# A half-filled token tile in two matmul passes instead of three, on one Trainium2 core

## The reference

```
kv = einsum('bhsd,bhse->bhde', k, v);  out = einsum('bhsd,bhde->bhse', q, kv)
x = out / sqrt(mean(out * out, -1) + 1e-6) * g_norm      # then heads side by side: (B, S, 512)
```

```
q, k, v = x @ wq[e], x @ wk[e], x @ wv[e];  a = softmax(causal(scale * q @ k.T))
ye = a @ v @ wo[e];  out += gate[e] * ye                 # gates: softmax over the top 2 of x @ w_gate
```

```
h = gelu_tanh(x @ w_in);  u, v = h[..., :512], h[..., 512:]
v_n = (v - mean(v)) / sqrt(var(v) + 1e-6) * g_ln
v_s = einsum('ts,bsd->btd', w_sg, v_n) + b_sg[None, :, None]
out = x + (u * v_s) @ w_out
```

## Time and profile before

| | |
|---|---|
| median of 3 runs | 925.42 us (923.89 to 925.64) |
| the profiled execution's own time | 923.37 us |
| its span, first to last instruction | 921.6 us |
| mean granted TensorE clock over it | 1.000 of full |
| busy: PE, PEld | 889.8 us (97%), 765.3 us (83%) |
| busy: DVE, ACT, POOL | 460.2 us (50%), 410.9 us (45%), 176.3 us (19%) |

### The profile page before, as it was taken

How to read it: one execution, slowest core, us unless ns; L and a number is a source line. 1 busy time by engine, 2 the same in 40 slices (tenths; PEclk the granted TensorE clock), 3 DMA queues, 4 the chain that set the end, 5 groups by cost and what they waited for, 6 DMA issues and landing times.

```text
span 921.6 us, 17530 instructions
## 1 busy us (share of the span) xinstructions
PE 889.8 (97%) x7009; PEld 765.3 (83%) x7009; DVE 460.2 (50%) x1218; ACT 410.9 (45%) x971; POOL 176.3 (19%) x209
## 2 busy tenths in 40 slices
PE   7699999999999999999999999999999999999897
PEld 3587898979888798978989789897988879897796
DVE  1667623475345743377334762347534574337730
ACT  0646523473335633365244652347333563336521
POOL 0400233003320033101330023300332003310230
DMA  9930303003030032100230030300303000000001
GB/s 278 268 62 2 97 8 94 10 2 104 6 98 2 1 104 60 44 2 22 84 87 18 1 101 4 95 9 2 104 7 97 2 2 1 20 33 1 1 1 52
DMA packets 77648, 45.76 MB, mean 50 GB/s; under 512 B 54592, under 2 KB 70976, under 8 KB 77568
## 3 DMA queue, kind: packets, MB, share of 16 engines
q1 hardware_dynamic: 77568, 44.63, 18.4%
HBM read 35.19 MB, written 9.44 MB: 48 GB/s over the span
## 4 chain that ended last, share of the span: by engine, by line
PE 81%; DVE 10%; ACT 7%; issue 1%; POOL 0%; DMA 0%; POOLq 0%; ACTq 0%; DVEq 0%
PE w L871 38%; PE t L871 19%; ACT probs L566 5%; PE t L925 4%; PE t L1013 4%; PE w L910 3%; DVE neg_max L686 3%; PE w L1058 3%; DVE probs L707 2%; PE t L941 2%; PE t L1002 2%; PE t L957 2%; PE w L978 2%; PE t L1021 2%; ACT work L579 1%; DVE yT L812 1%
## 5 line engine op out<-in xcount | busy, mean ns | idle before, releaser
L871 PE MATMUL w<-wout_s,big 128*128 128x512 f32 x480 | 119.2, 397 | 1.6 <-DVE big L735 1.6
L871 PE MATMUL w<-wsgT_s,big 128*128 128x288 f32 x768 | 110.8, 300 | 0.0
L871 PE MATMUL t<-big,wqk_s 128*128 128x288 f32 x768 | 109.6, 298 | 0.0
L871 PEld LDWEIGHTS w<-wsgT_s,big 128*128 128x128 f32 x768 | 103.3, 189 | 5.2 <-issue 5.2
L871 PEld LDWEIGHTS w<-wout_s,big 128*128 128x128 f32 x480 | 89.3, 188 | 22.0 <-DVE big L735 2.1
L871 PEld LDWEIGHTS t<-big,wqk_s 128*128 128x128 f32 x768 | 102.8, 188 | 0.4
L566 ACT ACTIVATE probs<-w,neg_max 128x64 f32<-128x64 f32 (+4 forms) x160 | 83.0, 525 | 44.5 <-DVE neg_max L686 44.5
L487 POOL TENSOR_TENSOR var_eps<-bn,eps_t 128x1 f32<-128x1 f32 x40 | 13.3, 333 | 445.6 <-DVE bn L723 444.9
L579 ACT ACTIVATE work<-t 128x384 f32<-128x384 f32 (+3 forms) x160 | 63.1, 448 | 44.5 <-PE t L925 44.1
L837 DVE SCALAR_TENSOR_TENSOR work<-w,gln_c,bias_t 128x576 f32<-128x576 f32 x32 | 26.2, 818 | 111.7 <-PE w L871 111.7
L600 ACT ACTIVATE big<-work 128x576 fp32r<-128x576 f32 x32 | 21.9, 686 | 133.1 <-POOL work L494 133.1
(11 more groups left out here) (104 smaller groups left out, 1417.2 us busy)
## 6 DMA issues: line engine op xcount, KB each, us to landing
kin<-in_k_dram SPq DMA_DIRECT2D x8, 1024.0 KB, 6.4
vin<-in_v_dram SPq DMA_DIRECT2D x8, 1024.0 KB, 9.5
qin<-in_q_dram SPq DMA_DIRECT2D x32, 256.0 KB, 4.8
out_dram<-work SPq DMA_DIRECT2D x32, 256.0 KB, 2.1
staged_win<-in_moe_w_in_dram SPq DMA_DIRECT2D x4, 512.0 KB, 5.7
probs<-in_moe_w_sg_dram SPq DMA_DIRECT2D x4, 288.0 KB, 4.1
kin<-in_k_dram SPq DMA_DIRECT2D x8, 128.0 KB, 3.2
vin<-in_v_dram SPq DMA_DIRECT2D x8, 128.0 KB, 7.4
```

What stands on the lines that cost most here:

```text
L871: last = nc.tensor.matmul(o, stationary(hs, c), mv(hm, c), start=c == of[0] and p == 0, stop=c == of[-1] and p == len(PASSES) - 1)
```

## The change

Where the first token tile is the stationary operand, its padding columns now hold the LO parts of the same 64 tokens (HI, columns 0 to 63). Two passes, (HI, HI) and (HI, LO), then give in result rows 64 to 127 the products of the high parts, and in rows 0 to 63 those of the low parts; the sum of the two halves is the product. ACT copies rows 0 to 63 down into partitions 64 to 127 (`low_v`, `low_h`, `low_out`), and DVE adds rows 64 to 127 to that. The four matmul groups lose their third pass.

With it go: DVE writes the LO part of tile 0 into the padding of HI, as an instruction of its own (in `xT`, `yT` and the gated tile `big2`); rows 0 to 63 of `vals` are set to zero once by POOL; an entry `low` for `h` 0 stands ahead of `h` 1 in the list, so that its sum is taken down at once, and `gelu` 0 works in place on the sum; and `h` 1 now takes the narrow buffers' turn, while `h` 2 goes to w1.

```diff
-    MLP = [("pv", N - 3), ("t", N - 2), ("h", 0), ("h", 1), ("scale", N - 1), ("t2", N - 2), ("gelu", 0), ("gelu", 1),
+    MLP = [("pv", N - 3), ("t", N - 2), ("h", 0), ("low", 0), ("h", 1), ("scale", N - 1), ("t2", N - 2), ("gelu", 0), ("gelu", 1),
-    H_SLOT = {1: "w1", 3: "w0", 4: "t1"}
+    H_SLOT = {2: "w1", 3: "w0", 4: "t1"}
...
+        low_v = sq_tile[:, 0:VW]
+        low_h = ln_tile[1]
+        low_out = probs[:, 0, 0, PAD:PAD + 512]
...
+                    elif U == ("v", 0):
+                        nc.scalar.activation(low_v[PAD:P, :], src(U)[0:PAD, 0:VW], ACT.Copy).then_inc(low_v_ready, 1)
                     elif kind == "v":
+                        if j == 1:
+                            u.wait_drained(act, part, i, ("v", 0))
+                    elif kind == "low":
+                        nc.scalar.activation(low_h[PAD:P, :], src(("h", 0))[0:PAD, 0:FF], ACT.Copy).then_inc(low_h_ready, 1)
                     elif kind == "gelu":
+                        if j == 0:
+                            u.wait_drained(act, part, i, ("h", 0))
+                            nc.scalar.activation(vg_tile[0][PAD:P, :], vg_tile[0][PAD:P, :],
+                                                 ACT.Gelu_apprx_tanh).then_inc(h0_summed, 1)
...
                 def gated_low(m):
-                    nc.vector.tensor_tensor(big2[:, LO, m, PAD:SP], gt_tile[m % 2], as_f32(big2[:, HI, m, PAD:SP]),
+                    nc.vector.tensor_tensor(big2[:, HI, m, 0:PAD], gt_tile[m % 2][:, 0:PAD],
+                                            as_f32(big2[:, HI, m, PAD:P]), ALU.subtract)
+                    nc.vector.tensor_tensor(big2[:, LO, m, P:SP], gt_tile[m % 2][:, PAD:S], as_f32(big2[:, HI, m, P:SP]),
                                             ALU.subtract).then_inc(gT_lo, 1)
...
+                        if j == 0:
+                            dve.wait_ge(low_v_ready, count(cur, 1, 1))
+                            give(nc.vector.tensor_tensor(vals[PAD:P, 0, :], ps[u.slot(part, U)][PAD:P, 0:VW],
+                                                         low_v[PAD:P, :], ALU.add), U)
...
+                            o = PAD if t == 0 else 0
+                            if t == 0:
+                                nc.vector.tensor_tensor(yT[:, HI, :, 0:PAD], x, hi, ALU.subtract)
+                            give(nc.vector.tensor_tensor(yT[:, LO, :, P * t + o:P * (t + 1)], x, hi, ALU.subtract), ("y", t))
...
+                    elif kind == "low":
+                        dve.wait_ge(low_h_ready, count(cur, 1, 1))
+                        give(nc.vector.tensor_tensor(vg_tile[0][PAD:P, :], ps[u.slot(part, ("h", 0))][PAD:P, 0:FF],
+                                                     low_h[PAD:P, :], ALU.add), ("h", 0))
...
+                    elif U == ("out_g", 0):
+                        dve.wait_ge(low_out_ready, count(cur, 1, 1))
+                        give(nc.vector.tensor_tensor(out_tile[0][PAD:P, :], ps[u.slot(part, ("out", 0))][PAD:P, 0:512],
+                                                     low_out[PAD:P, :], ALU.add), ("out", 0))
...
+                def passes_of(j):
+                    return ((HI, HI), (HI, LO)) if j == 0 else PASSES
                     elif kind == "v":
                         finish(split_product([dst(U)[:, 0:VW]], lambda h, c: xT[:, h, c, P * j:P * (j + 1)],
-                                             [lambda h, c: wv_s[:, h, c, :]], range(DC)), U)
+                                             [lambda h, c: wv_s[:, h, c, :]], range(DC), passes=passes_of(j)), U)
```

More of the change, by code:

```diff
@@ L175, in units @@
                     ring(("y", j // 2), NARROW[2:])
-            elif kind in ("split", "double", "exp", "scale", "gelu"):
+            elif kind in ("split", "double", "exp", "scale", "gelu", "low"):
                 pass
@@ L483, in body @@
                                          0.0).then_inc(big2_padded, 1)
+                        pool.wait_ge(w_lo, 3)
+                        nc.gpsimd.memset(vals[0:PAD, 0, :], 0.0).then_inc(vals_padded, 1)
                     elif kind == "h":
@@ L605, in body @@
                             act.wait_ge(stored[j % 2], count(cur, n_stored[j % 2], 16 + 16 * (j // 2)))
-                        give(nc.scalar.activation(out_tile[j % 2], x[:, 0:512], ACT.Copy), ("out", j))
+                        if j == 0:
+                            nc.scalar.activation(low_out[PAD:P, :], x[0:PAD, 0:512], ACT.Copy).then_inc(low_out_ready, 1)
+                        else:
+                            if j == 2:
+                                u.wait_drained(act, part, i, ("out", 0))
+                            give(nc.scalar.activation(out_tile[j % 2], x[:, 0:512], ACT.Copy), ("out", j))
                     if U in VHAT_AFTER:
@@ L781, in body @@
                         dve.wait_ge(xT_hi, count(nxt, NT, j + 1))
[L782 to L786, removed]
+                        o = PAD if j == 0 else 0
+                        x = ps[u.slot(part, U)][:, :].rearrange("p (c n) -> p c n", c=DC)[:, :, o:P]
+                        hi = as_f32(xT[:, HI, :, P * j + o:P * (j + 1)])
+                        if j == 0:
+                            nc.vector.scalar_tensor_tensor(out=xT[:, HI, :, 0:PAD], in0=x, scalar=gnorm_c[:, 0:1], in1=hi,
+                                                           op0=ALU.mult, op1=ALU.subtract)
+                        give(nc.vector.scalar_tensor_tensor(out=xT[:, LO, :, P * j + o:P * (j + 1)], in0=x,
+                                                            scalar=gnorm_c[:, 0:1], in1=hi,
+                                                            op0=ALU.mult, op1=ALU.subtract), U)
                         if to_scale is not None and j >= to_scale - 2:
@@ L811, in body @@
                             dve.wait_ge(yT_hi, count(cur, NT, t + 1))
[L812 to L815, removed]
+                            o = PAD if t == 0 else 0
+                            x = ps[u.slot(part, ("y", t))][:, 0:2 * P].rearrange("p (e n) -> p e n", e=EP)[:, :, o:P]
+                            hi = as_f32(yT[:, HI, :, P * t + o:P * (t + 1)])
+                            if t == 0:
+                                nc.vector.tensor_tensor(yT[:, HI, :, 0:PAD], x, hi, ALU.subtract)
+                            give(nc.vector.tensor_tensor(yT[:, LO, :, P * t + o:P * (t + 1)], x, hi, ALU.subtract), ("y", t))
                     elif kind == "t2":
@@ L861, in finish, with split_product @@
                     ins.then_inc(full[u.slot(part, unit)], 1)
-                def split_product(outs, stationary, movings, chunks, of=None, ready=None):
+                def split_product(outs, stationary, movings, chunks, of=None, ready=None, passes=PASSES):
                     of = of or chunks
@@ L1044, in body @@
                         finish(split_product([dst(U)[:, 0:512]], lambda h, c: yT[:, h, c, P * j:P * (j + 1)],
-                                             [lambda h, c: w2_s[:, h, c, FF:2 * FF]], range(EP)), U)
+                                             [lambda h, c: w2_s[:, h, c, FF:2 * FF]], range(EP), passes=passes_of(j)), U)
                     elif kind == "u":
@@ L1067, in body @@
                         split_product([dst(("out", j))[:, 0:512]], lambda h, c: yT[:, h, c, P * j:P * (j + 1)],
-                                      [lambda h, c: wo_s[:, h, c, :]], range(EP), of=range(EP + FC))
+                                      [lambda h, c: wo_s[:, h, c, :]], range(EP), of=range(EP + FC),
+                                      passes=passes_of(j))
                     elif kind == "out_g":
@@ L1075, in body @@
                                              [lambda h, c: wout_s[:, h, c - EP, :]], range(EP, EP + FC),
-                                             of=range(EP + FC)), ("out", j))
+                                             of=range(EP + FC), passes=passes_of(j)), ("out", j))
             body("pre", 0, None, (0, 0))
```

31 lines of the change are left out of this document (23 added, 8 removed).

## The result

The changed kernel took 930.05 us in the median of 5 runs (927.45 to 932.63), the kernel before 925.42 (923.05 to 926.20). The ratio is 1.0056, 95% interval 1.0035 to 1.0078. I had forecast 918.6 us, 912 to 924. The profiled execution took 927.45 us, 4.1 more than that of before, so the time is in the trace.

A forecast was written before the change was run, and what follows sets the result against it. PE (97% busy) was taken as the bound, each saving counting only up to PE's next wait. Seven batches at -0.91 and the last at -0.41 gave -6.8 us: 925.42 to 918.6 us, range 912 to 924.

The forecast's parts named there:

- The ceiling: All four shortened groups: matmuls removed, at 0.125 and 0.2325 us each, are worth at most 2.36 us a batch, 18.9 in all.
- `v`, -0.30 forecast: At `v` 2, which waits for DVE's sum of `v` 0: 0.30 of the 0.50 us a batch is kept.
- to 388.39, and 0.04 to PE: At `v` 2: DVE's sum of `v` 0 ends at 388.39 and PE starts 0.04 later, at 388.43.
- yT, -0.03: Tile 0 of yT: ACT's copy 0.11 shorter, DVE's two instructions 0.09 longer; bounds -0.1 and +0.15 a batch.
- Inner tiles, +0.76 forecast: `h` 1 waits for t2 and `pv` 8 for DVE's copies: 0.76 us a batch lost, bounds 0 and 1.2.
- `pv` 8 begins at 427.10: In the inner tiles: `pv` 8 waits for DVE's copies of `t2` 8, to 427.06, and begins 0.76 later than before.
- Output, -1.34 forecast: Output stage: `out_y` 0 saves 0.46 less 0.04 lost at `o` 0, `out_g` 0 saves 0.93; 1.34 to 1.35 a batch.
- PE starts at 462.72: 0.04 lost: At `o` 0: PE arrives at 462.68, ACT's first copy of `qT` is done at 462.68, so only 0.04 is lost.
- the eighth batch, where -0.84 was forecast: Output stage of the last batch: `out_y`'s saving is lost in PE's wait for DVE; -0.93 + 0.09 = -0.84.
- Covers: Slack hiding later work: 1.4 behind ACT's table load, 0.55 at `out_g` 0's low part, 0.38 at `x` 0.
- the four signs of being wrong: DVE's sum over 0.9 us, `h` 1 without a wait, `x` 0 waiting for scaling, or clock below 1.0 where PE waits longer.
- the one for "slower": Rival: half-height copies and sums on the way to `v` 2 and `pv` 8 cost twice the price; 935 us, chance 0.08.

The follow-up runs named there:

- the run at full height: The changed kernel with the copy and sum of `h` 0 over all 128 partitions without a shift; period 109.53 against 109.92, 926.69 us in one run.
- out alone: Two passes for tile 0 only in out_y and out_g, v and h as in the kernel before; median 918.61 us, ratio to before 0.9931.
- v 0 last: Two passes in v, out_y and out_g, h as before, and v 0 made the last of its four; median 914.12 us, ratio to before 0.9896.
- low late alone: The changed kernel with the entry low (sum of h 0) moved behind the copies of t2 8, buffers as in the changed kernel; 929.62 us, one run.

## Why the prediction was wrong, step by step

- **The ceiling and the places** were right: 0.125 and 0.2325 a matmul, and PE waits at `v` 2, `h` 1 and `pv` 8. A fourth wait, at `out_y` 1 for w1, was not named. The sign was wrong, since three terms were mis-sized, all to the good side: by 0.37, 0.57 and 0.33.
- **`v`, -0.30 forecast, +0.07 measured.** The step that failed is "to 388.39, and 0.04 to PE". ACT's copy came 0.14 later than read, since I took a start that overlaps the instruction ahead, and this one does not; the hand-over is 0.14 and not 0.04; and the matmuls behind it take 0.12 more than at their rate, which I had put at nothing. Together 0.36.
- **yT, -0.03, "taken as 0" but kept in the sum.** Right: exp's end to the next maximum is 0.69 after (405.46 to 406.15) against 0.73 before.
- **Inner tiles, +0.76 forecast, +1.33 measured.** The mechanism and its two waits stood. "`pv` 8 begins at 427.10" was 0.6 short: 0.39 is the overlap that the run at full height gave back, 0.20 that the hand-over to `pv` is 0.24 and not 0.04. The upper bound of 1.2 was too low.
- **Output, -1.34 forecast, -1.01 measured.** The failed step is "PE starts at 462.72: 0.04 lost". With 0.14 for the hand-over and 1.13 for `o` 0 behind a wait (0.89 without), the same chain in the kernel before gives 462.68 + 0.14 + 1.13 = 463.95 for `out_g` 0, against 464.03: 0.08 of `out_y`'s 0.46 could be kept, and not 0.42. `out_g`'s 0.93 came in full. In the eighth batch, where -0.84 was forecast, out alone gives -0.86: 915.9 - 811.82 = 104.08 from the last start to the end, against 921.6 - 816.66 = 104.94.
- **Covers** at ACT's table load, at `out_g` 0's low part and at `x` 0 held. None of the four signs of being wrong came in the loop: DVE's sum took 0.69, `h` 1 waited 1.36, `x` 0 did not wait, and the clock was 1.00.

Of the 1.27 us that the three terms missed, about 0.53 is lost overlap (0.14 and 0.39), 0.40 the hand-over (0.10, 0.20 and 0.10), and 0.36 the slow start behind it (0.12 and 0.24). The 0.04 from an engine's end to PE's start was taken from the hand-over to transposes. The earlier trace rows showed 0.14 ahead of `h` 1, and 1.65 for its 6 matmuls where 1.39 is the rate; I used neither. Of the rivals, the one for "slower" named the half-height instructions, but by their length, which was wrong; the cost is in their starts and in those of their followers.

## What to carry over

When PE is nearly full, a shortened stretch is worth its time only up to the next thing that PE waits for; take the distance from the last common event to the next product in both kernels (here 5.43 and 5.42) before counting matmuls. Each new wait on PE costs its hand-over and a slow restart besides the wait itself: 0.14 + 0.12 us at `v` 2, 0.14 + 0.24 at `o` 0, which is as much as two or three matmuls of 260 columns. A group whose result passes through two more engines belongs last among its equals, where no other waits for its buffer; made so, 0.37 us of the 0.50 counted. And an instruction that starts at another partition than its forerunners is not priced by its length alone: look in the trace at where such a one starts, and where the next does.

## What the runs showed of the hardware

The spread between runs of one kernel goes with TensorE's mean granted clock, which falls mostly in the preparation, in some profiled runs also near the end (with v 0 last to 0.83 from 890 to 900 us, with low late alone to 0.66 from 905 to 910). Of the run of out alone, two stretches of the view by windows (the stretch and its length, busy time and count of each engine, then the granted clock, DMA share and GB/s). The clock is 0.86 and 0.77 of full, a mix of the levels 2.4 and 1.2 GHz; from 60 to 900 us it is 1.00.

```profile
20.00:45.00 25.00, 18.93 (x173) 15.31 (x171) 15.67 (x19) 14.85 (x21) 9.42 (x12) 0.86 1.03 245
45.00:60.00 15.00, 13.21 (x78) 11.91 (x79) 9.70 (x13) 6.51 (x10) 1.20 (x4) 0.77 0.65 138
```

PE has long waits in the preparation, 1.45 and 2.10 us in the changed kernel, and its clock is 0.80 from 45 to 50 us and 0.82 from 50 to 54. The profiled run of the kernel before has the same waits (1.44 and 2.09) and 1.00 there, so the waits alone do not decide it. Runs of the kernel before beside one set of experiments took 922.92 to 923.63 us at a mean clock of 1.000 and 925.90 to 926.06 at 0.996; those of the changed kernel had 0.993 to 0.998. With out alone the runs at 1.000 took 915.30 and 915.42 us, those at 0.994 took 919.50 to 920.15. So 3 to 5 us of a difference between two single runs can be this, and the period does not contain it.
